# Where TensorE reads the tile bounds of eight experts: one by one between them, or all nine values ahead of the first tile

## The chip, the cores and the metric

The kernel runs on one core of a Trainium2 chip. A core has a matrix engine (TensorE, PE in the rows; its weight loads are PEld), a vector engine (VectorE, DVE), an activation engine (ScalarE, ACT), GpSimd (POOL) and SyncE (SP), each with an instruction queue of its own; a q behind an engine's name in a row means its sequencer. They wait for each other through semaphores only. The metric is the device time of one execution in microseconds.

## The reference, cut to what matters

Three layers follow one another: attention with four sink tokens and a sliding window, a gated feed-forward layer, and a routed mixture of eight experts over 1536 tokens of width 512. Only the third bears on the change:

```python
def _moe2_ref(x, w_skip, w_gate, w1, w2):
    do_compute = x @ w_skip > 0              # other tokens keep x
    xc = x[do_compute]
    logits = xc @ w_gate                     # 8 experts
    e_idx = np.argmax(logits, axis=1)
    gate_w = softmax(logits)[chosen]
    for e in range(8):
        h = np.maximum(xc[e_idx == e] @ w1[e], 0.0)
        y[e_idx == e] = gate_w * (h @ w2[e])
    out[do_compute] = xc + y
```

How many tokens an expert gets is known only once the routing is computed, on the chip.

## The kernel before, in words

**Staging.** Attention and the first feed-forward layer run with loops of fixed length. The last part of the first layer computes x1, one 128-token tile after the other, and routes it beside that: VectorE works out for each token an expert and a row in a buffer in DRAM (`expert_rows`), GpSimd scatters the rows there. Each expert's rows fill at least one row tile of 128. VectorE then makes `first_i`, nine integers in SBUF: the number of the first row tile of each expert and, as the ninth, their total (L1132); six instructions later it has `row_tile_i` and raises the semaphore `routed` (L1142). With the inputs used there are eleven row tiles, three more than experts.

**The expert stage, TensorE.** Its instructions stand in the `@block.tensor` function from L1446 on. `turn_rows(g)` waits for the rows of tile g (`rows_in`) and transposes them with four matmuls (L1451); ScalarE copies them to `xgT` (L801). Per expert, TensorE reads the end of its tile range with a `value_load` of one element of `first_i` (L1464), the beginning being the end of the one before, waits for w1, and runs a loop over the tiles.
**The other engines in it.** ScalarE evicts the two halves of the 64 matmuls with a ReLU into `hg_hi` (L807). VectorE makes `hg_lo`, the rest that `hg_hi` leaves (L1168). Before an expert's tiles, both split the w2 of the next expert into a high and a low part, in four quarters that arrive with two DMAs (ScalarE L763, VectorE L1087); ScalarE starts that only when the y matmuls of the tiles before the expert's are done (`y_in_psum`). VectorE then finishes the previous tile's result (`y_sb`, L1159) before it makes its `hg_lo`. GpSimd scatters `y_sb` to the output (L623) and, after the scatter has landed, fetches the rows of a later tile (L613); for tile 1 it first waits for the transposes of tile 0 (`xg_in_psum`). SyncE stores a tile of pad rows behind each expert's rows (L470, L471), and loads w1 (L432) and w2 (L440); these loads stand behind waits for the rows of certain tiles (`rows_in`): the w2 of expert 2 behind those of tile 1, the w2 of expert 3 behind those of tile 3.

**The first tile.** Its 128 rows don't come from `expert_rows`: GpSimd gathers them by index straight from the stored x1 (L600), as soon as the index is known. `turn_rows(0)` waits for that gather.

Every engine that loops over the tiles reads the bounds by itself: ScalarE and VectorE through `tiles` (L339).

Of the kernel before, what the change touches and what calls it, by code (L numbers as in the profile page):

```python
# [27 lines left out]
E, F2 = 8, 1024  # L28
# [5 lines left out]
MAXT = NT + E + 1  # L34
# [68 lines left out]
def build(nc, qT, kT, v, va, vb, sizes, w_gv, w_out, w_route, w1, w2, out):  # L103
    ctx = ExitStack()
    with ctx:
        def sb(name, shape, dt=F32):
            return ctx.enter_context(nc.sbuf_tensor(name, shape, dt))

        def sem(name):
            return ctx.enter_context(nc.semaphore(name))  # L110
# [127 lines left out]
        first_i = sb("first_i", [P, E + 1], I32)  # L238
# [70 lines left out]
        routed = sem("routed")  # L309
# [20 lines left out]
        def hold(engine, name):  # L330

            if name not in held:
                held[name] = sem(f"held_{name}")
            engine.sem_inc(held[name], 1)
# [496 lines left out]
        def _(d):  # L832
# [60 lines left out]
            for kind, tile, h, n in ORDER:  # L893
# [14 lines left out]
                elif kind == "T" and not on_act(kind, h):  # L908
                    d.wait_ge(pT_in_psum, n + 1)
                    if SBUF_USE[n] >= TURNED:  # L910
                        d.wait_ge(pv_done, SBUF_USE[n] - TURNED + 1)
                    nc.vector.tensor_copy(turned(probsT[:, SBUF_USE[n] % TURNED, :], qt), turned(pT_ps[n % 2][:, :], qt)
                                          ).then_inc(pT_by_dve, 1)
                elif kind == "Q":
                    d.wait_ge(probs_ready, tile * H + H)
                    nc.vector.tensor_scalar(rsum[:, tile % 2, :], sums[:, qt % 2, :], 1e-9, None, ALU.add
                                            ).then_inc(sums_step, 1)
                    d.wait_ge(sums_step, tile + 1)
                    nc.vector.reciprocal(rsum[:, tile % 2, :], rsum[:, tile % 2, :]).then_inc(rsum_ready, 1)
                elif kind == "X":  # L920
                    use = next(m for k, t, _, m in ORDER if k == "R" and t == tile)
                    d.wait_ge(pv_done, LAST_V[tile] + 1)
                    d.wait_ge(pT_by_act, evacuated(use)[1])
                    if tile >= 2:

                        d.wait_ge(xT_ready, tile - 1)
                    nc.vector.tensor_tensor(xT[:, tile % 2, :], o_ps[tile % 2][:, :], rbc_sb, ALU.mult
                                            ).then_inc(o_ready, 1)
                elif kind == "K":
                    make_mask(tile)  # L930
                    if tile == 0:
                        find_wide()
# [265 lines left out]
        def _(pe):  # L1198
# [248 lines left out]
            def turn_rows(g):  # L1447

                pe.wait_ge(rows_in, g * 16 + 16)
                for k in range(KD):  # L1450
                    last = nc.tensor.transpose(xg_ps[:, k * P:k * P + P], xg[:, k * P:k * P + P], ident[:, :])  # L1451
                last.then_inc(xg_in_psum, 1)

            pe.wait_ge(row_ready, NT + FREE_R)
            pe.sem_inc(h1_in_psum, DONE)
            pe.sem_inc(y_in_psum, DONE)

            turn_rows(0)
            pe.wait_ge(routed, 1)  # L1460
            end = 0
            for e in range(E):
                u = e % RING
                begin, end = end, pe.value_load(first_i[0:1, e + 1:e + 2], min_val=1, max_val=MAXT - 2)  # L1464
                pe.wait_ge(w1_in[u], 32 * (e // RING) + 32)
                hold(pe, "pe")
                with pe.Fori(begin, end) as g:
                    pe.wait_ge(xgT_ready, g + 1)
                    for half in range(2):

                        pe.wait_ge(hg_ready, g * 2 + half - 1 + FREE_H)
                        for f in range(FT2 // 2):
                            ps = hg_ps[half][:, f * P:f * P + P]
                            fc = slice((half * FT2 // 2 + f) * P, (half * FT2 // 2 + f + 1) * P)
                            for k in range(KD):
                                last = nc.tensor.matmul(ps, w1_sb[u][:, k, fc], xgT[:, k * P:k * P + P],  # L1476
                                                        start=(k == 0), stop=(k == KD - 1))
                        last.then_inc(h1_in_psum, 1)
                    turn_rows(g + 1)

                    pe.wait_ge(y_ready, g + 1)
                    for f in range(FT2):
                        if f % (FT2 // 2) == 0:

                            pe.wait_ge(piece_split, e * PIECES + f // (FT2 // 2) + 1)
                            pe.wait_ge(hg_ready, g * 2 + f // (FT2 // 2) + 1 + FREE_H)
                        hf = slice(f * P, f * P + P)
                        nc.tensor.matmul(y_ps[:, :], hg_hi[:, hf], w2_hi[u % 2][:, f, :], start=(f == 0), stop=False)  # L1488
                        nc.tensor.matmul(y_ps[:, :], hg_hi[:, hf], w2_lo[u % 2][:, f, :], start=False, stop=False)  # L1489
                        last = nc.tensor.matmul(y_ps[:, :], hg_lo[:, hf], w2_hi[u % 2][:, f, :],  # L1490
                                                start=False, stop=(f == FT2 - 1))
                    last.then_inc(y_in_psum, 1)
# [45 lines left out]
```

## Time and profile before

| | |
|---|---|
| median of 3 runs | 574.79 us (574.68 to 575.94) |
| the profiled execution | 575.94 us, of which the span of its instructions 574.4 |
| TensorE matmuls busy | 545.7 us, 95% of the span |
| VectorE, ScalarE, GpSimd busy | 242.6, 181.3, 96.8 us |
| the 64 matmuls per tile (L1476) | 704, 82.7 us, 280 ns each |
| DMA over the span | 73.84 MB, 129 GB/s |

A busy share says how much an engine does, not whether it sets the end; the chain of waits says that. It is followed back from the last instruction, at each step to what released it. The page cuts the span into 40 slices of 14.36 us; slice 29, counted from 1, covers the turn from routing to the first expert tile. Times in rows are microseconds from the start of the span; in the rows by line the durations are ns.

### The profile page before, as it was taken

What the parts mean: (1) busy time and instruction counts of PE and PEld (TensorE: products, weight loads), DVE (VectorE), ACT (ScalarE), POOL (GpSimd) and SP (SyncE); (2) the same over time, 40 slices, a digit from 0 to 9 for tenths busy, and PEclk for the clock granted to TensorE, in tenths of its full rate; (3) what the DMA queues carried; (4) which work ended last, traced back from release to release, by engine and by line L of the source; (5) the groups of instructions that cost most, each with busy time, mean ns of one, the idle gap of its engine ahead of it and who ended that gap; (6) DMA issues with size and microseconds to landing.
All of it is one profiled execution on the core that took longest, in us unless ns stands there. A gap on an engine that the chain in (4) does not pass through costs nothing.

```text
span 574.4 us, 10639 instructions
## 1 busy us (share of the span) xinstructions
PE 545.7 (95%) x3777; PEld 460.8 (80%) x3777; DVE 242.6 (42%) x686; ACT 181.3 (32%) x421; POOL 96.8 (17%) x137
## 2 busy tenths in 40 slices
PE   7899999999999999999999999999399999999994
PEld 5677777888888888888888888888288988899993
DVE  6777772323223333332333436543814144255311
ACT  4667772111101111111223334231313133244110
POOL 2233457201111110000000010101210101102111
PEclk9899999999999999999999999999689999999998
DMA  8988622210111111000071113651555786745111
GB/s 211 213 275 249 183 99 59 75 31 25 55 55 55 55 55 55 0 0 1 0 297 51 56 56 138 263 201 55 181 191 216 304 332 247 307 165 202 55 38 37
DMA packets 29591, 73.84 MB, mean 129 GB/s; under 512 B 2832, under 2 KB 15120, under 8 KB 25456
## 3 DMA queue, kind: packets, MB, share of 16 engines
q1 hardware_dynamic: 26592, 63.61, 32.7%
q0 software_dynamic: 2960, 9.73, 4.9%
q8 instruction: 23, 0.38, 0.3%
q14 instruction: 16, 0.13, 0.1%
HBM read 62.03 MB, written 11.29 MB: 128 GB/s over the span
## 4 chain that ended last, share of the span: by engine, by line
PE 78%; DMA 11%; DVE 4%; issue 3%; SPq 2%; ACT 1%; POOLq 0%; POOL 0%; DVEq 0%; ACTq 0%
PE bank L1279 11%; PE bank L1283 11%; PE bank L1281 11%; PE bank L1476 6%; PE bank L1356 6%; DMA w_raw<-w 6%; PE bank L1360 5%; PE bank L1358 5%; PE bank L1265 4%; PE bank L1242 3%; PE bank L1221 3%; PE bank L1488 2%; DMA out<-y_sb,idx_out 2%; PE bank L1490 2%; PE bank L1489 2%
## 5 line engine op out<-in xcount | busy, mean ns | idle before, releaser
L1279 PE MATMUL bank<-x_hi,w_hi 128*128 128x512 f32 x288 | 112.3, 390 | 0.3 <-issue 0.3
L1283 PE MATMUL bank<-x_hi,w_lo 128*128 128x512 f32 x288 | 112.1, 389 | 0.0
L1281 PE MATMUL bank<-x_lo,w_hi 128*128 128x512 f32 x288 | 112.1, 389 | 0.0
L1476 PEld LDWEIGHTS bank<-xgT,w_sb 128*128 128x128 f32 x704 | 82.4, 196 | 1.9 <-issue 1.2
L1476 PE MATMUL bank<-xgT,w_sb 128*128 128x128 f32 x704 | 82.7, 280 | 0.8 <-ACT xgT L801 0.8
L997 DVE TENSOR_TENSOR sig<-sig,bank 128x512 f32<-128x512 f32 x36 | 24.7, 687 | 127.0 <-ACT sig L703 127.0
L703 ACT ACTIVATE sig<-bank 128x512 f32<-128x512 f32 x36 | 21.5, 598 | 159.4 <-PE bank L1283 159.4
L1279 PEld LDWEIGHTS bank<-x_hi,w_hi 128*128 128x128 f32 x288 | 54.1, 188 | 11.7 <-issue 0.7
L1283 PEld LDWEIGHTS bank<-x_hi,w_lo 128*128 128x128 f32 x288 | 54.1, 188 | 11.3
L1281 PEld LDWEIGHTS bank<-x_lo,w_hi 128*128 128x128 f32 x288 | 54.1, 188 | 11.2
L1087 DVE TENSOR_TENSOR w_lo<-w_raw,w_hi 128x1024 fp32r<-128x1024 f32 x32 | 37.4, 1219 | 38.6 <-ACT w_hi L763 38.5
L1356 PE MATMUL bank<-wo_hi,hh_hi 128*128 128x512 f32 x132 | 53.6, 406 | 0.0
L1360 PE MATMUL bank<-wo_hi,hh_lo 128*128 128x512 f32 x132 | 51.7, 392 | 0.0
L1358 PE MATMUL bank<-wo_lo,hh_hi 128*128 128x512 f32 x132 | 51.4, 390 | 0.0
L661 ACT ACTIVATE probs<-scores_sb,negmax 128x208 f32<-128x208 f32 (+1 forms) x96 | 42.7, 446 | 21.8 <-DVE negmax L904 21.7
L763 ACT ACTIVATE w_hi<-w_raw 128x1024 fp32r<-128x1024 f32 x32 | 31.6, 1046 | 35.1 <-PE bank L1490 20.1
L585 POOL DMA_INDIRECT expert_rows<-x,row_i x12 | 11.7, 979 | 162.7 <-DVE row_i L1077 162.4
L1488 PE MATMUL bank<-w_hi,hg_hi 128*128 128x512 f32 x88 | 35.5, 403 | 2.1 <-DVE hg_lo L1168 2.1
L904 DVE CUSTOM_DVE_ANT_0 scores_sb<-bank,mask 128x208 f32<-128x208 f32 (+1 forms) x96 | 29.1, 357 | 17.7 <-PE bank L1221 14.5
L807 ACT ACTIVATE hg_hi<-bank 128x512 fp32r<-128x512 f32 x22 | 13.0, 591 | 67.9 <-PE bank L1476 67.9
L1490 PE MATMUL bank<-w_hi,hg_lo 128*128 128x512 f32 x88 | 34.4, 391 | 0.0
L1489 PE MATMUL bank<-w_lo,hg_hi 128*128 128x512 f32 x88 | 34.3, 390 | 0.0
(167 smaller groups left out, 731.2 us busy)
## 6 DMA issues: line engine op xcount, KB each, us to landing
w_raw<-w SPq DMA_DIRECT2D x16, 1024.0 KB, 7.6
w_sb<-w SPq DMA_DIRECT2D x16, 1024.0 KB, 6.5
w_raw<-w_gv SPq DMA_DIRECT2D x12, 512.0 KB, 3.5
va_sb<-v_long SPq DMA_DIRECT2D x10, 512.0 KB, 3.7
vb_sb<-v_tail SPq DMA_DIRECT2D x10, 320.0 KB, 4.8
xg<-expert_rows POOLq DMA_DIRECT2D x12, 257.0 KB, 3.0
q_sb<-qT SPq DMA_DIRECT2D x12, 256.0 KB, 5.0
k_sb<-kT SPq DMA_DIRECT2D x12, 256.0 KB, 5.9
```

Of the source, the lines that this page charges most:

```text
L661: nc.scalar.activation(probs[:, qt % 2, h * 2 + u, cols], scores_sb[:, i % 4, cols], ACT.Exp, bias=negmax[:, i % 4:i % 4 + 1], scale=-1.0, ...
L1087: last = nc.vector.tensor_tensor(w2_lo[u][:, f:f + FT2 // 4, :].rearrange("p k c -> p (k c)"), w2_raw[:, p, q:q + FT2 // 4, :].rearrange(" ...
L1279: nc.tensor.matmul(ps[:, :], w_hi[:, u, a, k, :], x_hi[:, k, tok], start=(k == 0), stop=False)
L1281: nc.tensor.matmul(ps[:, :], w_hi[:, u, a, k, :], x_lo[:, k, tok], start=False, stop=False)
L1283: last = nc.tensor.matmul(ps[:, :], w_lo[:, u, a, k, :], x_hi[:, k, tok], start=False, stop=(k == KD - 1))
L1356: nc.tensor.matmul(out_ps[u][:, :], h_hi, wo_hi[:, f, :], start=(f == 0), stop=False, skip_group_check=True)
L1358: nc.tensor.matmul(out_ps[u][:, :], h_hi, wo_lo[:, f, :], start=False, stop=False, skip_group_check=True)
L1360: last = nc.tensor.matmul(out_ps[u][:, :], h_lo, wo_hi[:, f, :], start=False, stop=(f == FT1 - 1), skip_group_check=True)
L1476: last = nc.tensor.matmul(ps, w1_sb[u][:, k, fc], xgT[:, k * P:k * P + P], start=(k == 0), stop=(k == KD - 1))
L1488: nc.tensor.matmul(y_ps[:, :], hg_hi[:, hf], w2_hi[u % 2][:, f, :], start=(f == 0), stop=False)
L1489: nc.tensor.matmul(y_ps[:, :], hg_hi[:, hf], w2_lo[u % 2][:, f, :], start=False, stop=False)
L1490: last = nc.tensor.matmul(y_ps[:, :], hg_lo[:, hf], w2_hi[u % 2][:, f, :], start=False, stop=(f == FT2 - 1))
```

## The change

TensorE waits for `routed` before it lets go of two semaphores and before `turn_rows(0)`, no longer behind it. Between that wait and `turn_rows(0)` it reads all nine values of `first_i` into nine registers. The loop over experts takes beginning and end from these registers; the eight `value_load`s in it are gone, and the first loop's beginning is now a loaded value where it was the constant 0. Nothing else differs, on no other engine.

```diff
             pe.wait_ge(row_ready, NT + FREE_R)
+            pe.wait_ge(routed, 1)
             pe.sem_inc(h1_in_psum, DONE)
             pe.sem_inc(y_in_psum, DONE)
 
+            first_of = [pe.value_load(first_i[0:1, e:e + 1], min_val=0 if e == 0 else 1, max_val=MAXT - 2)
+                        for e in range(E + 1)]
             turn_rows(0)
-            pe.wait_ge(routed, 1)
-            end = 0
             for e in range(E):
                 u = e % RING
-                begin, end = end, pe.value_load(first_i[0:1, e + 1:e + 2], min_val=1, max_val=MAXT - 2)
+                begin, end = first_of[e:e + 2]
                 pe.wait_ge(w1_in[u], 32 * (e // RING) + 32)
                 hold(pe, "pe")
                 with pe.Fori(begin, end) as g:
```

## Rows read from the trace of the kernel before

**Rows 1.** The page: TensorE's granted clock by slice, and the chain by engine.

```profile
PEclk9899999999999999999999999999689999999998
...
PE 78%; DMA 11%; DVE 4%; issue 3%; SPq 2%; ACT 1%; POOLq 0%; POOL 0%; DVEq 0%; ACTq 0%
```

**Rows 2.** Timeline around the first row tile: start, us, engine, line, idle before.

```profile
410.37 0.18 DVE L1142 TENSOR_TENSOR row_tile_i<-row_tile,real 128x21 int32<-128x21 f32 x1
...
412.95 1.11 PE L1451 MATMUL bank<-ident,xg 128*128 128x128 f32 x4 [5.95 <-DMA xg<-out,idx_first]
...
414.10 0.60 ACT L801 ACTIVATE xgT<-bank 128x512 f32<-128x512 f32 x1 [5.29 <-PE bank L1451]
...
414.83 1.43 PE L1476 MATMUL bank<-xgT,w_sb 128*128 128x128 f32 x5 [0.77 <-ACT xgT L801]
```

**Rows 3.** Loads of first_i: ns min/median/max, starts; whole run, then stretches.

```profile
L1464 PEldq TENSOR_LOAD <-first_i x8: 298/311/1358, 413.0 to 548.8; - x8
...
L1464 PEldq TENSOR_LOAD <-first_i x1: 310/310/310, 427.1 to 427.1; - x1
...
L335 PEldq EVENT_SEMAPHORE  x1: 51/51/51, 427.8 to 427.8; - x1
...
L339 ACTq TENSOR_LOAD <-first_i x1: 675/675/675, 410.6 to 410.6; - x1
...
L339 ACTq TENSOR_LOAD <-first_i x1: 946/946/946, 411.5 to 411.5; - x1
...
L1464 PEldq TENSOR_LOAD <-first_i x1: 649/649/649, 413.0 to 413.0; - x1
...
L335 PEldq EVENT_SEMAPHORE  x1: 51/51/51, 414.0 to 414.0; - x1
...
L1464 PEldq TENSOR_LOAD <-first_i x1: 1358/1358/1358, 509.6 to 509.6; - x1
```

**Rows 4.** Timeline of TensorE: the first matmuls of three row tiles.

```profile
430.93 0.83 PE L1476 MATMUL bank<-xgT,w_sb 128*128 128x128 f32 x6
...
500.39 7.31 PE L1476 MATMUL bank<-xgT,w_sb 128*128 128x128 f32 x64
...
513.46 0.72 PE L1476 MATMUL bank<-xgT,w_sb 128*128 128x128 f32 x5
```

**Rows 5.** Windows with L1476 alone: busy us and count, granted clock, DMA share, GB/s.

```profile
414.80:419.40 4.60, 4.57 (x21) 4.58 (x22) 0.50 0.94 271
419.50:424.10 4.60, 4.60 (x43) 4.60 (x43) 1.00 0.18 42
```

**Rows 6.** Timeline of TensorE: the transposes of tile 1.

```profile
424.95 0.66 PE L1451 MATMUL bank<-ident,xg 128*128 128x128 f32 x4 [0.51 <-DMA xg<-expert_rows]
```

**Rows 7.** Timeline of ScalarE and VectorE: the split of expert 2's w2.

```profile
431.30 2.00 ACT L763 ACTIVATE w_hi<-w_raw 128x1024 fp32r<-128x1024 f32 x2 [5.05 <-PE bank L1490]
...
432.39 2.36 DVE L1087 TENSOR_TENSOR w_lo<-w_raw,w_hi 128x1024 fp32r<-128x1024 f32 x2 [6.25 <-ACT w_hi L763]
...
435.82 2.36 DVE L1087 TENSOR_TENSOR w_lo<-w_raw,w_hi 128x1024 fp32r<-128x1024 f32 x2 [1.07 <-ACT w_hi L763]
...
438.10 0.74 DVE L1159 SCALAR_TENSOR_TENSOR y_sb<-bank,xres 128x512 f32<-128x512 f32 x1
```

**Rows 8.** The chain in order of time: start, us, what.

```profile
421.91 3.00 DMA xg<-expert_rows
...
425.36 9.35 DMA w_raw<-w
...
439.70 3.27 DMA out<-y_sb,idx_out
...
449.09 12.82 DMA w_raw<-w
...
480.70 7.76 DMA out<-y_sb,idx_out
...
494.42 0.33 PE bank L1451
```

## The prediction

> **What bounds the kernel now.** I read the page's chain of waits first: TensorE carries 78% of it, but the rest is not noise, since DMA carries 11% [rows 1]. So I looked at where the chain leaves TensorE, around the change. In the timeline of the turn from the second MoE's routing to its first row tile, TensorE has no work from 407.0 to 412.95: it waits 5.95 us for the gather of the first 128 rows. Its four transposes then start, ScalarE copies the result in 0.60, and the 64 matmuls of L1476 start at 414.83. VectorE's last routing instruction, the one that gives `routed`, ends at 410.37 + 0.18 = 410.55 [rows 2]. So between "first_i can be read" and "the gathered rows are there" lie only 2.4 us.
>
> The granted clock of that first tile is the lower level, 1.2 GHz, until about 419.5 (21 matmuls in 4.60 us), and the upper one, 2.4 GHz, after it (43 in 4.60) [rows 5]. It had fallen while TensorE was idle.
>
> From 408 to 494.4 the chain does not run through TensorE but through DMAs and the splitting of weights: pads, rows of tile 1 (421.91), w2 of expert 2 (425.36, 9.35 us), its split, the scatter of tile 0 (439.70), w2 of the next (449.09), and so on, until rows reach TensorE at 494.42 [rows 8]. After that TensorE is the bound: one row tile per 13.07 us (500.39 to 513.46) [rows 4], with no wait in it, to the end.
>
> **Removed: eight loads of a register between experts.** TensorE's queue has eight TENSOR_LOADs of first_i, of which the median takes 0.311 us and the longest 1.358 [rows 3]. The longest lies inside the tile period that takes 13.07 us all the same: the load starts at 509.6, while the matmuls behind it start at 513.46, so the sequencer was 3.9 us ahead of the array [rows 3, 4]. What hides them is the y matmuls already queued. The first of the eight (413.0 to 414.0 with its bookkeeping) lies beside ScalarE's copy, which ends at 414.70. Bounds: 8 x 0.66 = 5.3 us (a load with its bookkeeping, worked out below) if every one stood on the path, and 0. I take 0, since the longest of them left no mark on its period.
>
> **Moved: the wait for `routed`.** Alone it costs nothing: it is met at 410.55 and the gather lands at 412.95 [rows 2]. Two semaphore increments that now stand behind it are needed no earlier than the first tile's matmuls and results. Behind the wait on TensorE stand only the loads and the transposes.
>
> **Added: nine loads in one go, ahead of the first transposes.** Nothing is queued before them that could hide them, as TensorE is empty. One costs its TENSOR_LOAD and the bound check and bookkeeping: the load of 0.310 at 427.1 has the next instruction (the hold, L335) at 427.8, the one of 0.649 at 413.0 has it at 414.0; so about 0.35 comes on top of the load [rows 3]. That loads of one engine run one after the other is seen on ScalarE, whose second one starts at 411.5 when the first (410.6, 0.675) is over with its check [rows 3]. Nine undisturbed ones are 9 x 0.66 = 5.9 us. But in just this stretch loads take long: 0.675 and 0.946 on ScalarE and 0.649 on TensorE, against 0.31 [rows 3], which is 0.37 + 0.64 + 0.34 = 1.35 more if TensorE meets three such spells. Sum 7.3; from 410.6 the last ends at 417.9. Bounds: all nine undisturbed, 416.5; all nine at the mean of the three long ones (0.757 + 0.35 = 1.11), 420.6. I take 417.9, since the long ones all start by 413.0.
>
> *A rule against the change.* The Trainium skill ("DMA: Bandwidth & Descriptors", Latency and other measured facts) gives about 600 ns as the floor of a tensor_load. The trace here differs: 0.298 was the shortest on TensorE and 0.311 the median. By the page's figure an estimate would be 9 x 0.95 = 8.5 us, the last load over at 419.1, and some 1.2 us more than my sum.
>
> So the transposes start at 417.9 instead of 412.95: 4.9 us late. ScalarE's copy and L1476 follow with the same distance. For the clock I take the same 4.66 us at the lower level after the matmuls start; it may be a little less or more (below).
>
> **How much of the 4.9 reaches the end.** Two paths, and the later one counts.
>
> TensorE's own work: it waited 0.51 for the rows of tile 1 at 424.95 [rows 6], so it is 4.4 late after that. The five tile periods from 430.93 to 500.39 took 69.46, against 5 x 13.07 = 65.35 for undisturbed ones [rows 4]: 4.1 us of waits that a late TensorE would not notice. By this path 0.3 us is left.
>
> The weight chain: ScalarE starts the split of expert 2's w2 at 431.30, released by the last y matmul of tile 0, and its third quarter only when the second DMA has landed, at 425.36 + 9.35 = 434.71 [rows 7, 8]. With TensorE 4.4 late it starts at 435.7, when all of w2 has landed, and goes through without a pause. VectorE follows 1.09 behind it (432.39 - 431.30) and takes 1.14 per quarter (435.82 to 438.10 for two) [rows 7]; its tile result y_sb, queued behind them, starts at 435.7 + 1.09 + 4 x 1.14 = 441.35 instead of 438.10. That is 3.25 late: 4.4 less the 1.15 that ScalarE's pause for the DMA would have absorbed. From there everything in the chain hangs on what went before: y_sb, the scatter, the rows of tile 3, the w2 load behind them, its split, up to 494.42 [rows 8]; each moves by the same 3.25. hg_lo is queued behind y_sb on VectorE, so TensorE's y matmuls of tile 1 also come about 3.3 late, and the two paths agree there. After 494.42 there is no wait to absorb anything.
>
> What is not moved: the rows of tile 1 (421.91) need the first transposes done, on GpSimd's queue; they would be at 419.0, 2.9 us early enough. SyncE's loads beside mine may get slower; its pads would have to be over 3 us late before that showed, since TensorE is later than that already.
>
> **Sum.** The profiled execution took 575.94 (span 574.4, 1.5 around it): 575.94 + 3.25 = 579.2. It was the slowest of three; the median is 574.79, and I add the same 3.25: 578.1.
>
> **Rivals.**
> - *All nine loads long* (chance 0.10). Traffic on the DMA queues is heavy until 420, and the 1.358 one shows that a load can be worse [rows 3]. The last ends at 420.6, 7.65 late, less 0.5 and 1.15: 6.0, so 580.8. Against: TensorE's median is 0.31. The Trainium skill's figure from above, as an estimate, would end between this and my forecast, at 579.3.
> - *The clock stays low longer* (0.07). TensorE now idles 11 us rather than 6 before the transposes. If the lower level held twice as long after the matmuls start (9.3 us), 21 more matmuls would go at 0.219 instead of 0.107 [rows 5]: 2.3 us on top, 580.4. The other way, 3.2 us at that level instead of 4.66 gives 0.7 back.
> - *Hidden after all* (0.08; not slower). If back-to-back loads overlapped their checks, the nine would be done by 414.6, which is 0.44 each, and 1.65 us of delay is what the two absorptions above (0.5 and 1.15) take: 574.8. Against it is ScalarE's pair, which does not overlap.
> - *The collision at 480.70 goes* (0.06; not slower). The scatter there took 7.76 us, against 3.27 for the one at 439.70 [rows 8]. If, shifted against the weight loads, it were as short, the chain would win back 4.49, more than the 3.25, and TensorE's own 0.3 would decide: 575.1. It turns from the point where the scatter is issued clear of the weight loads. Against: those loads hang on the same chain and shift with it.
> - *The loop gains* (0.03, faster). If the removed loads did stand on the path, their 5.3 us would outweigh the 3.25: 572.7. Against it is the tile period with the 1.358 in it [rows 3, 4].
>
> **Numbers.** My forecast holds 0.66; its own range runs from 3.6 - 0.7 - 1.65 = 1.2 late (undisturbed loads, a short stretch at the lower clock; 576.0) to 4.7 late (579.5). About 0.2% (1.15 us) is what a measurement of this kernel can tell from no change, so every value of it is slower: 0.66 + 0.10 + 0.07 = 0.83. Same: 0.08 + 0.06 = 0.14. Faster: 0.03. The range over cases: 575.6 to 580.4.
>
> **What would show it.** In the profile after: nine TENSOR_LOADs from 410.6 on before L1451, the last over at about 417.9; the PE wait for the gather gone or put down to issue; L1476 starting near 419.8; ScalarE's four splits of w2 at about 435.7 without a pause; y_sb at 441.3; the tile period still 13.07. Wrong if the transposes start before 415, if y_sb of tile 0 stands at 438, or if the chain between 440 and 494 is shorter than before; and if the late tiles run under 13.07, the removed loads did cost something.

## The result and the profile after

The changed kernel takes 578.03 us (median of 6, 577.17 to 580.96), the one before beside it 574.11 (6 runs, 573.31 to 575.94): ratio 1.0075, 95% interval 1.0050 to 1.0099, so slower by some 4 us. The profiled execution took 580.38, with a span of 578.8; it is 2.35 above its median, that of before 1.83 above its own.

Single executions scatter by 3 us and more, part of it before the expert stage starts: L1142, the instruction that gives `routed`, starts at 410.37 in the profile before [rows 2] and at 409.54 in the one after. So I count times within the stage from the start of L1142.

The timeline of the changed kernel around its first row tile, which answers to [rows 2], and then its loads:

```profile
409.54 0.18 DVE L1142 TENSOR_TENSOR row_tile_i<-row_tile,real 128x21 int32<-128x21 f32 x1
...
418.29 1.11 PE L1451 MATMUL bank<-ident,xg 128*128 128x128 f32 x4 [12.11 <-issue]
...
419.44 0.60 ACT L801 ACTIVATE xgT<-bank 128x512 f32<-128x512 f32 x1 [11.47 <-PE bank L1451]
...
420.17 2.07 PE L1477 MATMUL bank<-xgT,w_sb 128*128 128x128 f32 x8 [0.77 <-ACT xgT L801]
```

By line (ns min/median/max, first and last start):

```profile
L1460 PEldq TENSOR_LOAD <-first_i x9: 297/549/930, 410.0 to 417.1; - x9
...
L1460 PEldq FUSED_REGOPS  x9: 146/146/167, 410.6 to 418.0; - x9
```

Nine loads stand between 410.0 and 418.2, one after the other, and the transposes start when the last is checked; TensorE's idle time before them is now put down to issue, not to the gather. Counted from L1142, the first of the 64 matmuls starts at 10.63 (420.17 - 409.54) instead of 4.46: 6.2 us late.

The granted clock of this tile, windows of L1477 alone (columns as in [rows 5]):

```profile
420.20:424.80 4.60, 4.60 (x21) 4.60 (x22) 0.50 0.20 57
...
425.00:429.60 4.60, 4.60 (x44) 4.60 (x42) 1.00 0.85 321
```

Again 21 matmuls in 4.60 us at 1.2 GHz, then 2.4 GHz: it moved along with the tile, and cost no more than before.

The timeline of ScalarE and VectorE on the w2 of expert 2, against [rows 7], and of TensorE behind them:

```profile
435.94 3.90 ACT L763 ACTIVATE w_hi<-w_raw 128x1024 fp32r<-128x1024 f32 x4 [5.00 <-PE bank L1491]
...
437.02 4.63 DVE L1087 TENSOR_TENSOR w_lo<-w_raw,w_hi 128x1024 fp32r<-128x1024 f32 x4 [5.52 <-ACT w_hi L763]
...
441.57 0.74 DVE L1159 SCALAR_TENSOR_TENSOR y_sb<-bank,xres 128x512 f32<-128x512 f32 x1
...
443.06 0.48 PE L1489 MATMUL bank<-w_hi,hg_hi 128*128 128x512 f32 x1
```

ScalarE's four quarters now go in one piece (x4), with no pause for the DMA: that pause was one of the waits that absorb a part of the delay. y_sb starts at 32.03 from L1142 instead of 27.73, 4.3 late, and TensorE's y matmuls of tile 1 follow without a wait.

Some of TensorE's later timeline, and then what it waited for in all of the stage:

```profile
483.56 0.50 PE L1489 MATMUL bank<-w_hi,hg_hi 128*128 128x512 f32 x1 [1.02 <-DVE hg_lo L1168]
...
496.29 0.64 PE L1451 MATMUL bank<-ident,xg 128*128 128x128 f32 x4
...
502.23 7.30 PE L1477 MATMUL bank<-xgT,w_sb 128*128 128x128 f32 x64
...
515.30 7.30 PE L1477 MATMUL bank<-xgT,w_sb 128*128 128x128 f32 x64
...
525.00 0.66 PE L1451 MATMUL bank<-ident,xg 128*128 128x128 f32 x4 [2.39 <-DMA xg<-expert_rows]
```

Waits of TensorE (us in total, times, longest):

```profile
PE bank L1451 <- issue: 12.1, 1, 12.1
...
PE bank L1451 <- DMA xg<-expert_rows: 2.4, 1, 2.4
...
PE bank L1489 <- DVE hg_lo L1168: 1.0, 1, 1.0
```

Two things differ from my picture. At 496.29 the rows are there in time, where TensorE waited 1.02 before: the chain has won back part of its delay. And at 525.00 there is a wait of 2.39 for rows, at a tile where the kernel before had none. The page's chain gives TensorE 85% now, against 78% [rows 1]:

```profile
PE 85%; DMA 5%; DVE 4%; issue 3%; ACT 1%; POOL 0%; POOLq 0%; DVEq 0%; SPq 0%; ACTq 0%
```

Starts of the first matmul of some row tiles, and the end of the span, all from L1142 on:

| kernel | tile 0 | 1 | 2 | 6 | 7 | 8 | end |
|---|---|---|---|---|---|---|---|
| before | 4.46 | 20.56 | 34.70 | 90.02 | 103.09 | 116.17 | 164.0 |
| after | 10.63 | 26.02 | 39.10 | 92.69 | 105.76 | 121.43 | 169.3 |
| late by | 6.17 | 5.46 | 4.40 | 2.67 | 2.67 | 5.26 | 5.3 |

So 3.5 of the 6.2 us are absorbed by tile 6, and then 2.6 come on top.

### The profile page after: what moved, and what is told of

Read it like the earlier page. It is cut to its first block, busy times and chain, and to the rows that moved or that the text cites. A ratio compares the mean times of both kernels' runs of the same rounds, so it can differ in the third digit from the quotient of the medians.

```text
span 578.8 us, 10642 instructions
## 1 busy us (share of the span) xinstructions
PE 544.3 (94%) x3777; PEld 460.3 (80%) x3777; DVE 242.7 (42%) x686; ACT 181.0 (31%) x421; POOL 96.4 (17%) x137
## 4 chain that ended last, share of the span: by engine, by line
PE 85%; DMA 5%; DVE 4%; issue 3%; ACT 1%; POOL 0%; POOLq 0%; DVEq 0%; SPq 0%; ACTq 0%
PE bank L1279 11%; PE bank L1283 11%; PE bank L1281 11%; PE bank L1477 10%; PE bank L1356 6%; PE bank L1360 6%; PE bank L1358 6%; PE bank L1265 4%; PE bank L1242 3%; PE bank L1489 3%; PE bank L1491 3%; PE bank L1490 3%; PE bank L1221 2%; DMA w_raw<-w 2%; PE bank L1376 2%
## 5 line engine op out<-in xcount | busy, mean ns | idle before, releaser
L1477 PEld LDWEIGHTS bank<-xgT,w_sb 128*128 128x128 f32 x704 | 82.4, 196 | 1.9 <-issue 1.2
L1477 PE MATMUL bank<-xgT,w_sb 128*128 128x128 f32 x704 | 82.7, 280 | 0.8 <-ACT xgT L801 0.8
```

## The experiments

**1. The wait alone, and three loads.** e1 moves only the wait; e2 reads three values ahead and six in the loop.

```diff
e1:          pe.sem_inc(y_in_psum, DONE)
+            pe.wait_ge(routed, 1)
             turn_rows(0)
-            pe.wait_ge(routed, 1)
             end = 0
e2: as e1, and
+            first_of = [value_load of first_i[e] for e in range(3)]
             turn_rows(0)
...
-                begin, end = end, pe.value_load(...)
+                begin, end = end, first_of[e + 1] if e + 1 < len(first_of) else pe.value_load(...)
```

> Only the wait for routed is moved ahead of the first transposes; the eight loads stay in the loop, one per expert. My theory: the wait is met 2.4 us before the gathered rows arrive, so nothing moves; the first L1451 starts with the landing of the gather (some 2.4 us after routed) and the time is that of before, within 0.2% (ratio 0.998 to 1.002). Rival, the wait itself costs (a late wake-up, the two increments behind it): 1 us or more of the 4 us appears.

> Three values (for the first two experts) are read ahead of the first transposes, the other six in the loop. My theory: a read costs 0.66 us undisturbed and some 1.0 in this stretch, so the third is over about 2.8 to 3.3 us after routed, 0.4 to 0.9 us after the gather; the transposes start that much late, and the waits of TensorE and of the weight chain (0.5 and 1.15 us in the profile before) absorb it: ratio 0.999 to 1.002. Rival, each load costs in proportion: a third of the change's 4 us, 1.3 us, ratio 1.0023.

e1: 575.08 against 575.36, ratio 0.9988 (0.9972 to 1.0004). e2: 574.69, ratio 0.9987 (0.9967 to 1.0007). TensorE's first transposes, and in e2 the loads ahead of them:

```profile
412.55 1.09 PE L1451 MATMUL bank<-ident,xg 128*128 128x128 f32 x4 [5.69 <-DMA xg<-out,idx_first]
```

```profile
413.33 1.11 PE L1451 MATMUL bank<-ident,xg 128*128 128x128 f32 x4 [6.69 <-issue]
```

By tensor (ns min/median/max, first and last start; us to landing where it is a DMA):

```profile
L1460 PEldq TENSOR_LOAD <-first_i x3: 652/691/734, 410.2 to 412.3; - x3
```

In e1 the transposes still wait for the gather, so the moved wait costs nothing. In e2 they start by the loads (idle put down to issue), and the first matmuls start 5.22 from L1142, 0.8 later than before; nothing of it is left at the end (164.1 against 164.0). The three loads take 0.65 to 0.73 us each. A third of the loads does not cost a third: that would be a ratio of 1.0023, and the interval of e2 ends at 1.0007.

**2. The nine behind the transposes.** e3 waits for `routed` and loads only after `turn_rows(0)`.

```diff
+            turn_rows(0)
+            pe.wait_ge(routed, 1)
             first_of = [nine value_loads]
-            turn_rows(0)
```

> All nine loads stand behind the first transposes instead of ahead of them; the wait for routed is between. My theory: the loads then start with the transposes, 2.4 us later than in the changed kernel, and take 6 to 7.5 us, since the worst spell of long loads is over; the first L1477 waits for them instead of for ScalarE's copy (1.9 us), so it starts 9 to 10 us after routed, 0.8 to 1.6 us earlier than the 10.64 of the changed kernel. Ratio to before 1.003 to 1.007. Rival, only the delay of the transposes and of the rows behind them counts, not that of the first matmuls: ratio 1.000.

578.39, ratio 1.0050 (1.0031 to 1.0070): as expected, and nearly the price of the change. The transposes wait for the gather, and the loads then hold up the first matmuls:

```profile
412.93 1.11 PE L1451 MATMUL bank<-ident,xg 128*128 128x128 f32 x4 [5.48 <-DMA xg<-out,idx_first]
...
420.82 1.43 PE L1477 MATMUL bank<-xgT,w_sb 128*128 128x128 f32 x5 [6.77 <-issue]
```

By tensor (ns min/median/max, first and last start; us to landing where it is a DMA):

```profile
L1461 PEldq TENSOR_LOAD <-first_i x9: 296/363/897, 412.9 to 419.7; - x9
```

L1477 starts at 10.01 from L1142, though the transposes are not late. So what counts is when the first tile's matmuls start. The profiled execution of e3 took 582.49, 4.1 above its median; it also has the wait of 2.4 us at tile 8 that the changed kernel showed.

**3. The changed kernel again, and with the transfers kept apart.** In the changed kernel the rows that arrive late at 525 are issued 0.5 us behind the last expert's w2; in the one before, 0.5 us ahead of it. e4 is the changed kernel once more; e7 gates that w2 in the changed kernel, e8 in the one before.

```diff
e7, e8:      for e in range(2, E):
+                if e == E - 1:
+                    sp.wait_ge(rows_in, 9 * 16)
                 load_w2(e)
```

> The changed kernel once more. I expect a ratio of 1.005 to 1.009. The first profile of it waited 2.39 us for rows at 525 that the kernel before did not wait for, and it was 2.4 us above its own median. If that wait is part of the change, it stands in this profile too; if it is a collision of transfers that comes and goes, this profile ends about 2.7 us later than the one before, counted from routed, with the surplus of the tile periods elsewhere.

> The changed kernel, but SyncE issues the w2 of the last expert only when the rows of tile 8 have landed. In both profiles of the changed kernel these rows are issued 0.5 us behind that w2 and take 5.2 us, in the one of before 0.5 us ahead of it and take 3.0. My theory: the late start pushes the rows behind the w2; gated, they land in 3 us and TensorE's wait of 2.4 there goes: ratio to before 1.001 to 1.004 instead of 1.006. Rival, the wait only moves to another tile or the w2 comes too late: ratio as with the change, 1.005 or more.

> The same gate in the kernel before. If the collision is one that comes and goes in executions of the kernel before too (they scatter from 573 to 579), the median falls by up to 1 us: ratio 0.997 to 1.000. If it is only there with the late start: 1.000.

e4: 578.78 against 575.36, ratio 1.0058 (1.0035 to 1.0080). e7: 578.76 against 575.62, ratio 1.0051 (1.0036 to 1.0065). e8: 575.71, ratio 1.0000 (0.9989 to 1.0012). SyncE's and GpSimd's issues in the kernel before, the time to landing of the rows behind them:

```profile
517.29 2.60 SPq L440 DMA_DIRECT2D w_raw<-w  x2
...
516.81 0.55 POOL L613 DMA_DIRECT2D xg<-expert_rows  x1 [7.85 <-issue]
```

By tensor (ns min/median/max, first and last start; us to landing where it is a DMA):

```profile
DMA to landing us min/median/max: 3.0/3.0/3.0
```

and in the changed one:

```profile
519.13 2.60 SPq L440 DMA_DIRECT2D w_raw<-w  x2
```

A piece of the chain (start, us, what):

```profile
519.64 5.32 DMA xg<-expert_rows
```

in e7, whose SyncE holds the w2 back, by tensor:

```profile
L615 POOL DMA_DIRECT2D xg<-expert_rows x1: 553/553/553, 519.7 to 519.7; - x1
...
DMA to landing us min/median/max: 3.0/3.0/3.0
```

and the waits of TensorE in e4, the wait for rows among them:

```profile
PE bank L1451 <- DMA xg<-expert_rows: 2.3, 1, 2.3
```

With the gate the rows are back at 3.0 us and the wait is gone: tile 8 starts at 118.85 in e7, 13.07 after tile 7, and the span ends at 166.7, against 169.3 and, in e4, 168.8. But over all timed executions e7 is hardly better than e4; its profiled one lies at its median (578.63), while the two profiles of the changed kernel lie 1.8 and 2.35 above theirs. e12 below, which is not late, has the wait in its profile too, and so has e3: these four profiled executions lie 1.8 to 4.1 above their medians, the ten others from 0.2 below to 1.8 above. So I infer that the wait comes and goes and that the median holds little of it; no trace shows an execution of the changed kernel itself without it. In the four, the rows are issued 0.3 to 0.8 us behind the w2 and land in 5.1 to 5.6 us. My expectation of 1.001 to 1.004 was wrong: I took the profile for the typical execution. In the kernel before the gate changes nothing (e8).

**4. More of it: eighteen ahead, nine in the loop, two in the loop.**

```diff
e5:          first_of = [nine value_loads]
+            first_of = [nine value_loads]
             turn_rows(0)
e6, e12:         begin, end = end, pe.value_load(...)
+                for at in range(E):        # e12: range(1)
+                    pe.value_load(first_i[0:1, at + 1:at + 2], min_val=1, max_val=MAXT - 2)
```

> Eighteen loads ahead of the first transposes: the nine of the change, twice (the first nine results unused). My theory: serial loads on an empty engine, each 0.66 to 0.9 us; the transposes start 15 to 16 us after routed instead of 8.7, so 6.5 us later than in the changed kernel, and since what absorbs (about 3 us) is used up by the first nine, nearly all of that shows: ratio to before 1.015 to 1.019. The rows of tile 1 then also wait for the transposes, on GpSimd. Rival, the price of the change is the collision at 525 that any small delay brings on, not the delay itself: ratio 1.006 to 1.009, as with nine.

> The kernel before with eight more loads at each expert, between the loop's own load and the wait for w1: nine loads, 6 us, eight times over. My theory: loads between experts are hidden while they fit into what TensorE's sequencer is ahead of its array (3.9 us in the profile before), so one costs nothing and nine cost 6 - 3.9 = 2 us at each of the seven borders after the first, plus 5 us at the first: part of it absorbed by the waits until 494, so 8 to 18 us in all, ratio 1.015 to 1.03. Rival one, a load in the loop costs its time in full: 8 x 5.3 = 42 us, ratio 1.07. Rival two, the loop's loads are free whatever their number: the first border's 4 us alone, ratio 1.006.

> The kernel before with one load more at each expert, so two in the loop instead of one. Nine there cost 29 us. My theory: what counts is what the sequencer is ahead of the array, 3.9 us; two loads are 1.3 us and fit, so the ones that the change removes were free: ratio 0.999 to 1.002, and tile periods of 13.07 where they were. At the first border they stand beside ScalarE's copy (1.9 us from the transposes on) and cost at most 0.3. Rival, each load in the loop costs 0.4 to 0.5 us, as 29 us over 64 loads would have it: 8 x 0.45 = 3.6 us, ratio 1.006.

e5: 584.38 against 575.62, ratio 1.0177 (1.0142 to 1.0212), from four runs.

```profile
424.60 1.11 PE L1451 MATMUL bank<-ident,xg 128*128 128x128 f32 x4 [17.39 <-issue]
...
426.48 3.75 PE L1479 MATMUL bank<-xgT,w_sb 128*128 128x128 f32 x16 [0.77 <-ACT xgT L801]
```

By tensor (ns min/median/max, first and last start; us to landing where it is a DMA):

```profile
L1460 PEldq TENSOR_LOAD <-first_i x9: 308/449/924, 411.1 to 418.1; - x9
...
L1462 PEldq TENSOR_LOAD <-first_i x9: 300/301/307, 418.8 to 424.0; - x9
```

The first matmuls start 15.90 from L1142, 5.3 later than in the changed kernel, and the medians rise by 5.3 (3.4 over before for nine in e4, 8.8 here). What absorbs is used up by the first nine: at tile 6 e5 is 8.2 us late (98.23), so it has won back 3.2 of its 11.4, and the changed kernel 3.5 of its 6.2. The second nine, from 418.8 on, take 0.301 each; the first nine, in the traffic of the pads and rows, have a median of 0.449. The busy share of the DMA engines is 0.99 from 411.0 to 418.5 and 0.23 from 418.8 to 424.3. My expectation had the transposes at 15 to 16 us from `routed`; they start at 14.0, as the second nine are short.

e6: 605.09, ratio 1.0512 (1.0491 to 1.0533), 29.5 us, where I had 8 to 18. e12: 575.71 against 576.23, ratio 0.9991 (0.9977 to 1.0005). What TensorE waited for in each:

```profile
PE bank L1478 <- issue: 22.8, 8, 6.6
```

```profile
PE bank L1478 <- issue: 1.7, 1, 1.7
...
PE bank L1451 <- DMA xg<-expert_rows: 3.8, 2, 2.5
```

By tensor (ns min/median/max, first and last start; us to landing where it is a DMA):

```profile
L1466 PEldq TENSOR_LOAD <-first_i x8: 294/296/720, 414.4 to 552.6; - x8
```

Nine loads outlast what the sequencer is ahead: TensorE stands at every border (8 waits, 22.8 us, the longest 6.6 at the first, the others 2.2 to 2.5). About 4.4 us of smaller waits that the kernel before has behind its gather are gone in return. The rest is the clock, which I had not counted: behind the border at 469.8 it is 0.65 for 4.6 us, its mean over the execution is 0.958 against 0.981, and the matmuls are busy 556.5 us against 545.7, 10.8 longer. Two loads show one wait for issue, 1.7 us, at the first border, where they don't fit beside ScalarE's copy (the first matmuls start at 4.97 from L1142, 0.5 late); that is absorbed. The later borders have none. So a second load in the loop is free, and with it the one of the kernel before. That is a load added; no run takes the eight out of the loop without putting them elsewhere.

**5. The clock.** Filling transposes of the identity, whose results nobody reads, in the time in which TensorE has nothing to do: e9 in the changed kernel, e10 in the one before.

```diff
+            def fill(n):
+                for i in range(n):
+                    nc.tensor.transpose(xg_ps[:, i % 4 * P:i % 4 * P + P], ident[:, :], ident[:, :])
e9:  +       fill(16) ahead of the wait for routed, fill(4) behind each of the nine loads
e10: +       fill(24) ahead of turn_rows(0)
```

> The changed kernel with filling transposes of the identity into the unused bank while TensorE has nothing to do: 16 before the wait for routed and 4 behind each of the nine loads, so that the clock does not stay at the lower level. They compute nothing that is used. If the clock rises before the first tile, its 64 matmuls take 7.2 us instead of 9.6, the late start falls from 6.2 to 3.8 us at the end of them, and by the sum with two absorptions 4.3 us late becomes some 2: ratio 1.002 to 1.004. Rival, the end hangs on the start of the first tile alone and not on its pace: ratio as with the change, 1.005 to 1.008.

> The kernel before with 24 such transposes while it waits for the gather. My theory: up to 494 the weight chain and the rows set the end of the kernel before, not TensorE, so 2.4 us saved on the first tile are waited for later: ratio 0.999 to 1.001. Rival, TensorE sets it: ratio 0.996.

e9: 576.44 against 575.21, ratio 1.0023 (1.0009 to 1.0037). e10: 575.12, ratio 1.0007 (0.9993 to 1.0022). TensorE's first tile in e9 and in e10, the latter with the transposes of tile 1 behind it:

```profile
419.90 7.41 PE L1487 MATMUL bank<-xgT,w_sb 128*128 128x128 f32 x64 [0.77 <-ACT xgT L801]
```

```profile
413.93 7.41 PE L1481 MATMUL bank<-xgT,w_sb 128*128 128x128 f32 x64 [0.77 <-ACT xgT L801]
...
425.07 0.66 PE L1451 MATMUL bank<-ident,xg 128*128 128x128 f32 x4 [3.73 <-DMA xg<-expert_rows]
...
481.34 0.50 PE L1493 MATMUL bank<-w_hi,hg_hi 128*128 128x512 f32 x1 [1.70 <-DVE hg_lo L1168]
```

Both run the tile's 64 matmuls in 7.41 us, at the upper level (2.4 GHz). In e9, which starts it as late as the changed kernel does (10.69), the price falls from 3.4 (e4) to 1.2 us, by as much as the tile is quicker (9.64 in the changed kernel, 7.41 here). In e10 nothing is gained: TensorE waits 3.73 for the rows of tile 1, where it waited 0.51 [rows 6], and 1.70 for VectorE at 481. And the clock falls again behind that longer wait. The window, columns as in [rows 5] with the busy times of VectorE, ScalarE and GpSimd ahead of the clock:

```profile
426.30:429.20 2.90, 2.90 (x8) 2.30 (x7) 0.00 (x0) 0.07 (x1) 0.73 (x2) 0.50 0.86 325
```

The matmuls with w2 take 0.63 us there instead of 0.39, so tile 1 starts at 22.46 from L1142, 1.9 later than before (20.56), and that too is gone by tile 6 (89.79 against 90.02). That is the asymmetry of the kernel before: TensorE early is worth nothing, TensorE late is worth what exceeds its waits.

**6. A shorter chain.** In e11 GpSimd stores the pads of experts 5 to 7 while it waits for its scatter.

```diff
SyncE:   for e in range(E):   ->   for e in range(5):
GpSimd, between issue and wait of its last scatter (its waits for the pads follow suit, not shown):
...
+        for e in range(5, E):
+            filled = pool.value_load(count_i[0:1, e:e + 1], min_val=0, max_val=NTOK)
+            pool.dma_start(expert_rows[bass.ds(filled + e * CAP, P), :], pad[:, :]).then_inc(pool_padded, 16)
```

> The kernel before, but the pad rows of experts 5 to 7 are stored by GpSimd, while it waits for its scatter, and not by SyncE; the last pad lands some 3 us earlier than 420.2, so the rows of tile 1 and the w2 of expert 2 behind them come 2 to 3 us earlier. My theory of a chain that starts with the pads: everything up to 494 moves 1 to 3 us ahead, as far as TensorE's own work allows (its waits there sum to 4 us): ratio 0.995 to 0.998. Rival, the reads and stores on GpSimd's queue take as long as they do on SyncE's (1.1 us each and more), or the transfers wait for each other: ratio 1.000, or above.

574.68 against 575.21, ratio 0.9991 (0.9974 to 1.0008): not told apart from no change, where I had expected 0.995 to 0.998. SyncE's last pad is issued some 3 us earlier than before (413.1 against 416.6) and GpSimd's three at 410.0, 411.4 and 413.2, but the rows of tile 1 are issued no earlier, here the timeline of GpSimd:

```profile
421.51 0.54 POOL L624 DMA_DIRECT2D xg<-expert_rows  x1 [5.84 <-DMA xres<-expert_rows]
```

By tensor (ns min/median/max, first and last start; us to landing where it is a DMA):

```profile
L472 SPq DMA_DIRECT2D expert_rows<-pad x5: 332/333/345, 407.9 to 413.1; - x5
...
L613 POOL DMA_DIRECT2D expert_rows<-pad x3: 542/572/592, 410.0 to 413.2; - x3
```

before, the same transfer was issued at 421.9 [rows 8]; from L1142 on both are 11.54. The last pad, in the chain of the kernel before and then in that of e11:

```profile
416.56 3.64 DMA expert_rows<-pad
```

```profile
413.15 6.90 DMA expert_rows<-pad
```

Issued 3.4 us sooner, it takes 3.3 longer to land. That the transfers of pads and rows wait for each other, my rival, fits this; what they wait for the runs don't show. None of these versions beats the kernel before.

## Why the prediction was right

**The removed loads are free.** Right: the tile periods in the changed kernel are the same 13.07 (502.23 to 515.30), and one load more per border (e12) costs nothing. e6 shows where that ends.

**The moved wait is free.** Right, shown by e1.

**Nine loads ahead of the transposes.** The mechanism was right, the size short: I had 7.3 us from 410.6 on, three of the nine long. They took 8.2, with a median of 0.549: five of them took 0.55 to 0.93, and the last of these started at 417.1, where I had taken the long ones to start by 413.0. They also began 0.25 later after `routed` than I had taken from ScalarE's. So the delay of the first matmuls was 6.2 instead of 4.9, between my sum and the bound "all nine long" (7.65). The estimate by the Trainium skill ("DMA: Bandwidth & Descriptors", Latency and other measured facts), with 600 ns a load, was 6.2 late. It is close here only: outside that stretch, in e5's second nine, a load took 0.301, half of that.

**The clock.** Right: 4.6 to 4.7 us at the lower level in both. e9 shows what I had not priced in the sum, that the lower clock on this tile becomes worth its full time once TensorE is late.

**What is absorbed.** I had 0.5 (rows of tile 1) and 1.15 (ScalarE's pause). Measured are 0.7 (6.17 late at tile 0, 5.46 at tile 1) and 1.2 (5.47 late at the start of ScalarE's split, 4.30 at y_sb): right in kind and near in size. e2 and e10 show the absorption from both sides, e5 shows that it ends.

**"From there each moves by the same 3.25": the last transfer broke it.** The delay in the chain was 4.3 at y_sb and still 4.0 when GpSimd issued the rows of tile 6, here before and then after:

```profile
490.21 0.55 POOL L613 DMA_DIRECT2D xg<-expert_rows  x1 [8.49 <-issue]
```

```profile
493.40 0.55 POOL L613 DMA_DIRECT2D xg<-expert_rows  x1 [8.64 <-issue]
```

These are 79.84 and 83.86 from L1142. But the rows took 4.16 to land in the kernel before (490.21 to 494.37) and 2.8 in the changed one:

```profile
DMA to landing us min/median/max: 2.8/2.8/2.8
```

So they landed only 2.7 late, just as TensorE came to them with its own work at 496.29. The scatter ahead of them took as long as at 480.70 [rows 8]; L623 by line (ns min/median/max, first and last start):

```profile
L623 POOL DMA_INDIRECT out<-y_sb,idx_out x1: 1020/1020/1020, 483.7 to 483.7; - x1
...
DMA to landing us min/median/max: 7.9/7.9/7.9
```

So something of the rival "the collision goes" did come, on the rows and not on the scatter. In e4 tile 6 is 2.4 late (92.39) by another way: the rows are issued 2.9 late and land in 3.64. So the two profiles of the changed kernel and that of e7 (92.70) agree on 2.4 to 2.7 late at tile 6, but not on the way there; why the chain loses a part of its delay on the way stays open. In exchange the profile has the wait at tile 8, which I did not foresee.

**Luck in the number.** Two errors of size nearly cancel: 1.3 us too little delay at the start, and 1.6 us too much kept between y_sb and tile 6 (4.30 to 2.67). The medians say 3.9 beside the first runs of before, 3.4 in e4 and 3.1 in e7; I had 3.25. So the path was right, and that the number comes so close is in part luck. For the profiled execution, 575.94 + 3.25 = 579.2 was predicted and 580.38 measured: counted from L1142 it is 5.3 late, the 2.6 at tile 8 included, and it reached L1142 0.8 sooner. Two numbers of the prediction are loose: the 4.7 at the upper end of "its own range" is not worked out, and the range of 575.6 to 580.4 leaves out the times of four of its rivals.

**The rivals.** Hidden after all: fallen (the first matmuls start at 10.63 from L1142, where it would have been 6.1). A longer low clock: fallen, the first tile took 9.64 us against 9.62. All nine long: five of nine. The loop gains: fallen, by e12 and the periods.

## What to carry over

Reading a value into a register with its bound check cost TensorE 0.65 us here (nine of them from 418.8 to 424.5 in e5), and more while pads and rows were moving, but only where nothing was queued ahead of it. Between full tiles it is hidden behind queued work; pulled together ahead of the first instruction of a stage, nine of them are serial and stand in the open. Before hoisting something out of a loop, ask what covers it where it is and what would cover it where it goes; and when a late start looks absorbed by waits, count the waits, since they pay only once.

## What the runs showed of the hardware

- A TENSOR_LOAD took 0.300 to 0.307 us on TensorE with the DMA engines 0.23 busy (nine in e5), and up to 0.93 in the stretch of pads and row transfers, where they were 0.97 busy (changed kernel, 410.0 to 418.3); FUSED_REGOPS stayed at 0.146 to 0.167. The longest, 1.358, at 509.6 in the kernel before, also fell in busy transfers (1.01 from 509 to 511). Single ones of 0.30 stand in the busy stretch too.
- Between experts TensorE's sequencer hid two loads with their checks (e12: no wait at the seven later borders) but not nine (e6: 2.2 to 2.5 us at each of them), where the clock also fell behind the borders.
- Behind a wait of TensorE of 3.73 us the granted clock fell to 0.50 (1.2 GHz) from 426.3 to 429.2 (e10); behind one of 0.51 at the same place it stayed at 1.00 from 425.0 to 430.9 (before).
- The same 257 KB of rows landed in 3.0 us issued 0.5 us ahead of the w2, two loads of 1 MB (before), in 5.3 us issued 0.5 us behind it (after), and in 3.0 us with it held back (e7).
